# Layer one of an mLSTM and two-MoE kernel in five groups of two or three units, with two units ahead of it in place of three

## The reference

```python
m_new = np.maximum(f_gate[:, :, t] + m, i_gate[:, :, t])
f_stab, i_stab = np.exp(f_gate[:, :, t] + m - m_new), np.exp(i_gate[:, :, t] - m_new)
C = f_stab * C + i_stab * outer(v, k);  n = f_stab * n + i_stab * k
y = sigmoid(o_gate) * (C @ q) / np.maximum(np.abs(n . q), 1.0)
```

## Time and profile before

| | |
|---|---|
| median of 3 runs | 929.63 us (929.35 to 931.27) |
| the profiled execution, its own time | 928.55 us |
| its span | 926.7 us |
| PE busy | 917.5 us (99%) |
| VectorE, ACT, POOL busy | 622.0, 435.9, 621.6 us |
| mean granted clock | 0.996 |

### The profile page before, as it was taken

The page is one execution under the profiler, slowest core; times in us unless marked ns, Lnnn a source line. Parts: engine busy times, 40 slices in busy tenths (PEclk is TensorE's granted clock), DMA queues, the critical chain, the costliest instruction groups (busy, mean ns, idle before and its releaser), DMA issues.

```text
span 926.7 us, 16315 instructions
## 1 busy us (share of the span) xinstructions
PE 917.5 (99%) x6081; PEld 904.5 (98%) x6081; DVE 622.0 (67%) x1194; ACT 435.9 (47%) x887; POOL 621.6 (67%) x639
## 2 busy tenths in 40 slices
PE   9899999999999999999999999999999999999998
PEld 7799999999999999999999999999999999999998
DVE  7767555557867887866666666666666666666665
ACT  4544434326664444545445454444454444444442
POOL 5875454643877667677777767777776777677652
PEclk9899999999999999999999999999999999999999
DMA  9824204201111111111111111121111112111102
GB/s 291 254 65 114 71 26 115 78 1 38 37 38 38 38 37 39 38 38 40 57 39 52 38 38 37 38 60 38 52 37 38 38 38 56 42 51 39 37 2 86
DMA packets 28238, 53.54 MB, mean 58 GB/s; under 512 B 2288, under 2 KB 16224, under 8 KB 27776
## 3 DMA queue, kind: packets, MB, share of 16 engines
q1 hardware_dynamic: 27008, 46.73, 17.5%
q10 hardware_dynamic: 1152, 5.77, 1.6%
HBM read 50.45 MB, written 2.05 MB: 57 GB/s over the span
## 4 chain that ended last, share of the span: by engine, by line
PE 93%; DMA 2%; DVE 2%; SPq 1%; issue 0%; ACT 0%; POOL 0%; DVEq 0%; POOLq 0%
PE bank L1659 36%; PE bank L1636 33%; PE bank L1516 9%; PE bank L1526 6%; PE bank L1530 3%; PE bank L1441 2%; DMA rw<-rows 1%; PE bank L1376 1%; PE bank L1435 1%; DMA factors<-dec 1%; PE bank L1414 1%; PE bank L1548 1%; SPq L425 1%; PE bank L1431 0%; DVE acc L1277 0%
## 5 line engine op out<-in xcount | busy, mean ns | idle before, releaser
L1636 PE MATMUL bank<-xo,wu 128*128 128x384 f32 (+1 forms) x1792 | 377.4, 338 | 0.7 <-DVE s L1297 0.5
L1636 PEld LDWEIGHTS bank<-xo,wu 128*128 128x128 f32 (+1 forms) x1792 | 306.6, 188 | 1.4 <-DVE s L1297 0.7
L1281 DVE SCALAR_TENSOR_TENSOR acc<-bank,prob,acc 128x320 f32<-128x320 f32 x336 | 184.7, 550 | 143.2 <-PE bank L1659 141.7
L1659 PE MATMUL bank<-wd_hi,h_hi 128*128 128x320 f32 x768 | 232.7, 311 | 0.1
L1659 PE MATMUL bank<-wd_lo,h_hi 128*128 128x320 f32 x768 | 231.3, 309 | 0.0
L741 POOL TENSOR_TENSOR h_lo<-r,h_hi 128x384 fp32r<-128x384 f32 x192 | 194.5, 1032 | 52.4 <-ACT r L691 52.3
L741 POOL TENSOR_TENSOR wu<-raw_up,wu 128x512 fp32r<-128x512 f32 (+1 forms) x128 | 145.6, 1168 | 103.9 <-ACT wu L499 98.6
L690 ACT ACTIVATE h_hi<-c 128x384 fp32r<-128x384 f32 x192 | 100.3, 522 | 185.4 <-DVE c L1303 142.0
L1659 PE MATMUL bank<-wd_hi,h_lo 128*128 128x320 f32 x768 | 174.9, 309 | 0.0
L1659 PEld LDWEIGHTS bank<-wd_lo,h_hi 128*128 128x128 f32 x768 | 145.0, 189 | 0.0
L1659 PEld LDWEIGHTS bank<-wd_hi,h_hi 128*128 128x128 f32 x768 | 144.7, 188 | 0.2
(11 more groups left out here) (148 smaller groups left out, 1309.4 us busy)
## 6 DMA issues: line engine op xcount, KB each, us to landing
raw_up<-ups SPq DMA_DIRECT2D x32, 512.0 KB, 3.5
raw_down<-downs SPq DMA_DIRECT2D x32, 320.0 KB, 2.9
rw<-rows SPq DMA_DIRECT2D x12, 480.0 KB, 7.7
qk_s<-qk SPq DMA_DIRECT2D x12, 416.0 KB
fb<-factors SPq DMA_DIRECT2D x9, 512.0 KB, 6.4
m_raw<-up_down ACTq DMA_DIRECT2D x2, 1440.0 KB, 9.7
result<-acc SPq DMA_DIRECT2D x12, 160.0 KB, 1.8
decb<-factors SPq DMA_DIRECT2D x18, 80.0 KB
```

The source lines that it names most:

```text
L1281: ins = stt(acc[:, unit, :], bank_, prob[:, unit, ex:ex + 1], acc[:, unit, :], ALU.mult, ALU.add)
L1636: last = mm(ring_bank(q, b), a, m, start=(i == 0 and k in (0, 1, 4)), stop=(i == len(parts) - 1), skip_group_check=True)
L1659: last = mm(ps_t[n % RING][:, 0:DM], h[half + f][:, cols], w_[w][:, f, :], start=(i == 0), stop=(i == len(parts) - 1))
```

## The change

The groups of layer one become 2, 2, 2, 3 and 3 units (`SIZES`). Only units 0 and 1 are made ahead of it; units 2 and 3 are made in group 0, 4 and 5 in group 1 (one in seven steps, `PERIODS`), 6 to 8 in group 2 and 9 to 11 in group 3 (one in five). `unit_at(g, step, f)` tells which unit has which stage in step f. Unit 2 gets its factors and decays by DMA, as the later ones: `spread_decays`, `copy_decb`, the tensor `select` and the second `turn_factors` go. `fg`, `first_f` and `dec` move into the memory of the last weight tables, so VectorE's two waits go; ACT waits instead, ahead of piece 8 (`TABLES = 8`). In group 0 `gact` isn't used: the max is written over the hidden tile in its bank, of which there are three then. The weights come in six DMAs, the last three issued later, and three pieces stand ahead of group 0, the others one in each step.

```diff
-UNIT = 5
-EARLY = 6
+SIZES = (2, 2, 2, 3, 3)
+PERIODS = (7, 7, 5, 5)
+STEPS = {7: (0, 1, 2, 4, 5, 7, 8, 9), 5: (0, 1, 2, 3, 4, 5, 6, 7)}
+SCORE, QUERY, WEIGH, HEADS, DENOM, OUTPUT, TURN, LOW = range(8)
+READY = 2
-TABLES = 12
-LOADS = (0, 2, 6, 11, FT1)
-LATE = {2: (6, 7), 3: (8,), ...}
+TABLES = 8
+LOADS = (0, 2, 4, 6, 9, 12, FT1)
+LEAD = 3
...
+    def hidden_bank(g, f):
+        n = tokens(g)
+        return ((bank[6], bank[7], bank[5])[f % 3] if g == 0 else ps_h[f % 2])[:, 0:n]
+
+    def activated(g, f):
+        return hidden_bank(0, f) if g == 0 else gact[:, f % 2, 0:tokens(g)]
...
             turn_factors()
             gates_exp(1)
             load_weights(0)
-            turn_factors(1)
+            act.wait_ge(rows_in[1], 16)
             load_weights(1)
...
             def mlp_piece_at(f):
-                for q in LATE.get(f, ()):
+                q = f + LEAD
+                if q == TABLES:
+                    act.wait_ge(f_stored, 32)
+                    act.wait_ge(dec_stored, 32)
+                    act.wait_ge(iT_ready, len(PARTS))
+                    act.wait_ge(dE_ready, 2)
+                if q < FT1:
                     mlp_piece(q)
+                if f in (1, 4):
+                    load_weights({1: 4, 4: 5}[f])
...
-            turn_lo(xa_hi, 2, ps_turn_of[2], 2 * P, xa_ready)
-            decays(1, 0, 0)
-            dve.wait_ge(f_stored, 32)
-            dve.wait_ge(dec_stored, 32)
...
+                    for j in range(2):
+                        if f >= j and unit_at(g, SCORE, f - j) is not None:
+                            u = unit_at(g, SCORE, f - j)
+                            if u != STARTS[g + 1] or g == 0:
+                                decays(u, j)
+                    if g + 2 < G and f >= FT1:
+                        decays(STARTS[g + 2], f - FT1)
...
+                        if g == 0 and f >= 3:
+                            pe.wait_ge(lo1, f - 2)
+                        if g > 0 and f >= 2:
                             pe.wait_ge(g1, s - 1)
-                        first_product(ps_h[f % 2], f, ...)
+                        first_product(hidden_bank(g, f), f, ..., STARTS[g] * P, n, wait_x_lo).then_inc(h1, 1)
```

More of the change, by code:

```diff
@@ L38 @@
 PARTS = ((0, P), (P, 2 * P), (2 * P, S))
-EARLY = 6
+SIZES = (2, 2, 2, 3, 3)
+G = len(SIZES)
+STARTS = tuple(sum(SIZES[:g]) for g in range(G))
+PERIODS = (7, 7, 5, 5)
+STEPS = {7: (0, 1, 2, 4, 5, 7, 8, 9), 5: (0, 1, 2, 3, 4, 5, 6, 7)}
+SCORE, QUERY, WEIGH, HEADS, DENOM, OUTPUT, TURN, LOW = range(8)
+READY = 2
 SLOTS = 2
@@ L73, in after, with tokens, unit_at, factor_loads @@
     return m + (FREE + 1)
-def same_slot(i):
-    return (1, 3, 2)[i]
+def tokens(g):
+    return SIZES[g] * P
+def unit_at(g, step, f):
+    if g + 1 == G:
+        return None
+    for i in range(SIZES[g + 1]):
+        if i * PERIODS[g] + STEPS[PERIODS[g]][step] == f:
+            return STARTS[g + 1] + i
+    return None
+def factor_loads(u):
+    return (u - READY) // GT + 1
 NEG = -1e30
-def build(nc, gates, select, qk, rows, up_down, rest, ups, downs, wgate, consts, factors, out):
+def build(nc, gates, qk, rows, up_down, rest, ups, downs, wgate, consts, factors, out):
     f32, f32r = mybir.dt.float32, mybir.dt.float32r
@@ L205, in build @@
     mark[0] = after_x + TABLES * PM * 4
+    fg = sb("fg", [GH, S])
+    first_f = sb("first_f", [GH, S])
+    dec = sb("dec", [GH, S])
     ig = sb("ig", [GH, S])
@@ L443, in _ @@
             sp.dma_start(cst[:, :], consts).then_inc(consts_in, 16)
[L444 to L450, removed]
+            for u in range(READY):
+                load_qk(u, u)
+                load_rows(u, u)
+            load_qk(READY, READY)
+            load_rows(READY, READY)
             sp.wait_ge(f_ready, 2)
@@ L1515, in first_product, with second_product @@
                         wait_x_lo()
-                    last = mm(dst[:, 0:GN], w, x, start=(i == 0), stop=(i == len(parts) - 1))
+                    last = mm(dst, w, x, start=(i == 0), stop=(i == len(parts) - 1))
                 return last
-            def second_product(f, slot, first, last, hi, lo, wait_lo, done, wait_bank=None):
+            def second_product(f, size, slot, first, last, hi, lo, wait_lo, done, wait_bank=None):
                 col = f * PM + 2 * P
                 for w in (hi, lo):
-                    for t in range(GT):
+                    for t in range(size):
                         if first and w is hi and wait_bank is not None:
```

499 lines of the change are left out of this document (217 added, 282 removed).

## The result

The changed kernel takes **932.53 us** (median of 10 runs, 932.01 to 935.08), the kernel before, run beside it, 930.19 (10 runs). The ratio is 1.0026, with a 95% interval of 1.0014 to 1.0037: slower by 2.3 us, a little more than the 1.9 us that I named as the bound of what can be told from no change. The range held it, but the case that I gave the best chance (no difference, +0.95 us, 927.8 to 931.5) did not come. The profiled execution took 932.21 us with a span of 930.4, 3.7 us over that of before (928.55 and 926.7).

What follows compares the result with a forecast made beforehand. PE, busy in 99% of the span, was taken as the bound. The terms -7.2 - 3.7 + 4.95 + 1.4 + 2.8 + 2.2 + 0.5 gave +0.95 us on the median 929.63, so 930.6 us, range 924.0 to 936.5.

Steps and rivals of the forecast that it cites:

- the case that I gave the best chance: Whole kernel: gains and losses nearly balance, +0.95 us, 930.6 us, between 927.8 and 931.5; chance 0.36.
- Step 1: Start ahead of layer one: only two units made there, first product at about 23.8 in place of 30.96, -7.2 us.
- Step 2: Group 0: VectorE's wait on the table stores goes, and with it all 3.7 us of standing, -3.7 us.
- Step 3: Group 0: unit 2 is made there, where PE is full, +4.95 us.
- Step 4: Groups of two: first-product matmuls of 256 columns at 0.121 us each, 384 replacing 256 of 0.176, +1.4 us.
- Step 5: Group 0: PE stands for POOL's weight pieces, thirteen inside the shorter group at 1.95 us each, +2.8 us.
- Step 6: Changes of group: VectorE's max, scans and low part delay its copies; PE stands 1.2, 0.8 and 0.2, +2.2 us.
- Step 7: Group 2, three units in shorter steps: weights 0.2 to 0.4 us late for the heads twice, +0.5 us.
- third case: Group 0: POOL's weight pieces bound it, 934.5 us, last group's first product at 218; chance 0.27.
- The rival of 0.147: First-product matmuls: 256 columns cost as much as 320, 10 us more, 940.6 us; chance 0.04.
- The slower one: POOL's weight pieces bound group 0, 3 to 4 us longer, a lower clock can add; 934.5 us, chance 0.27.

Runs made afterwards that it cites:

- Run 5: Kernel before with fg, first_f and dec behind eight weight pieces and VectorE's wait on their stores gone: 930.28 us against 931.22, ratio 0.9994.
- run 6: As Run 5, with the fourth weight load issued in step 0 of group 0: 930.62 us against 931.22, ratio 0.9991.
- run 1: Changed kernel with VectorE's two scans at a change of group moved into steps 0 and 1 of the next group: 932.96 us, ratio 1.0031.
- run 12: run 9 with the scan left at the group's end held until POOL's last low part is done: 929.78 us against 930.75, ratio 0.9993.
- Run 8: Changed kernel with outputs in step 6 and a fourth weight piece made ahead of the layer: 931.35 us, ratio 1.0008.
- run 7: Changed kernel with the low part of the rest of pieces 3 to 15 made by no engine (part of result differs): 931.69 us, ratio 1.0008.
- run 9: Run 8 with one of the two scans at the group's end, the other in step 0 of the next: 930.19 us against 930.74, ratio 0.9993.
- run 3: Changed kernel with outputs and their copy in step 6 in place of 7 in groups that make two units: 931.99 us, ratio 1.0021.
- run 2: Changed kernel with the low part of the 128-row rest of pieces 3 to 15 given from POOL to VectorE: 943.95 us, ratio 1.0142.
- run 4: Changed kernel with the edits of run 1, run 2 and run 3 together: 946.69 us, ratio 1.0156.
- run 10: Run 8 with groups of two, three, two, two and three units: 945.81 us, ratio 1.0161.

## Why the prediction was right and wrong

The groups' lengths and the rows give an account that can be laid beside the prediction's sum. Work by rows is 48 steps of 1.82, 16 of 2.73 and ten units of 4.95, with 3.2 for turns and late columns: 183.8 us of the 194.67 (the 3.2 are 0.6 in group 0 and 0.87 for turns in each of the three others). Before it was 178.8 of 182.52. So the change added 5.0 of work, took 3.7 of standing away and put 10.9 there.

| Step of the prediction | predicted | measured in the profile |
|---|---|---|
| 1. start | -7.2 | -8.1 |
| 2. wait on the stores | -3.7 | -3.7 |
| 3. one more unit in the layer | +4.95 | +4.95 (taken, see below) |
| 4. 256 columns | +1.4 | 0.0 |
| 5. standing in group 0 | +2.8 | +5.1 |
| 6, 7. standing in groups 1 to 3 | +2.7 | +5.8 |
| last group's start | +0.95 | +4.0 |

The sum was too low by 5.4 us in the two rows of standing, and too high by 2.3 in the start and the 256 columns. That leaves 3.1 us in the account, and 1.9 in the time, since the forecast was laid on a median that is 1.1 us above the profiled execution. So that the range held 932.53 is in part luck: the standing was forecast at half of what it was, and other misses made up for part of it. The last group's start at 217.49 is near the 218 that the prediction gave for its third case.

- **Step 1** held: heads of unit 1 at 15.15 (predicted 15.4), first product at 22.82 (23.8). Unit 1's output ends at 21.15 (21.7), and the product follows 1.7 later (2.1 to 2.4). The long scan of `dec` takes 1.16 us where it took 2.60, with POOL no longer busy beside it. What I named only as a risk went the other way: eight of the change's ten runs have a mean clock of 1.000, and in the profiled one it stayed at 1.00 through this start, where before it fell at 24 us and, by the mean clock of most of its runs, for longer. How much of the 8.1 us the clock gave isn't measured.
- **Step 2** held in the account of the two profiles and is mis-sized by itself. Runs 5 and 6 made this part alone and it brought 0.4 to 0.9 us, with intervals that include no gain. Run 5 shows what the clamp's wait covered: PE's own wait for unit 3's keys and queries, which land at the same time with or without it. A step that I never wrote is that the profiled execution's start stands for the others. It was among the best: of the 98 runs of the kernel before beside runs 1 to 12, four had a clock of 0.996 or more, and one was faster than the profiled one. This is why the profiles differ by 3.7 us and the medians by 2.3.
- **Step 3** isn't measured by itself, and no kernel without the unit's work was tried. That group 3 has no standing, and is 59.42 long, which is 43.7 + 14.85 + 0.87, speaks for the 4.95.
- **Step 4** was mis-sized: 0.117 us a matmul, near the straight line (0.118). The fixed part that I kept for 0.121 isn't there. The Trainium skill's 262 cycles for 256 columns (TensorE: Matmul & The Clock Gate, Back-to-back issue gap) would be 0.109; the row decides. The rival of 0.147 is refuted.
- **Step 5** had the right engine and the wrong place. I had reckoned by POOL's sum of work, with piece 15 as the late one. POOL ended 0.6 us later than I said, and piece 15 was in time. The waits are at pieces 3, 4, 10 and 11, where ScalarE's rounding, a unit's stages and a meeting with a scan come together. I had taken 1.95 a piece, for fewer meetings; three small subtractions took 0.93 to 0.97 us more than alone, ahead of these waits. Run 8 removed all four waits by one piece more ahead, run 7 two of them by taking 8.8 us of subtractions. Beyond the 2.9 us of waits, each stop costs more than its idle time, which was in no term (below). With this, five stops (0.27 each) and one wait for a copy (0.3) make 4.6 of the 5.1 us; the rest isn't placed.
- **Step 6** was right in its mechanism at the first change (1.2 predicted, 0.88 in the row) and blind to the other half: the same scans hold POOL's low part, 0.82 us at the second change. The rule that I quoted for step 5 (the Trainium skill, GPSIMD Engine Reference, 1. Specifications) covers this case as well, a VectorE instruction with two SBUF inputs beside POOL, and I applied it to the pieces alone. Runs 9 and 12 show both halves: -1.1 and -0.7 in group 1.
- **Step 7** (+0.5) has 0.9 us in two waits ahead of heads in group 2. The profile names no releaser; VectorE's weights end 0.2 us ahead of both, so late weights are likely. Not foreseen were waits for ScalarE's last 64 columns before the turn of a unit (0.3 to 0.4, one in each of groups 0 to 2), which run 3 took away in groups 0 and 1.
- **The rivals.** The slower one had the right sign and cause, POOL's pieces, at 934.5, and gave the clock as what could add to it. In the change the clock did the reverse: it stayed up; in runs 2, 4 and 10 it did what the rival said. The measured time lies midway between 930.6 and 934.5. Balance was forecast since I summed the standing place by place and priced only the chains that I looked at.

## What to carry to other kernels

When a stage is filled by one engine and its steps get a third shorter, every chain through the other engines that used to be hidden comes out, one place at a time; look for them at each place where a transfer of work between engines was "just in time", and not at the engine's total. Removing one such wait pays only in part (of the 1.7 us of waits taken away in run 1, 0.4 arrived in the profile and 0.7 in the time at 1.000), and moving work to an engine with idle time can cost far more than it frees: run 2 lost 11.4 us where I had hoped for a gain of 2.5. Before a start-up stretch is priced from one profile, see whether that execution is a typical one.

## What the runs showed of the hardware

- **VectorE's scan and POOL's instructions hardly run side by side, and the delay goes in both directions.** In most rows the one that starts first goes at full speed and the other waits: `m_st` took 1.42 in place of 0.45 beside a scan that started 0.05 us earlier. A scan that starts while POOL is busy waits, and at times POOL's next instruction goes ahead of it too: the scan took 3.69 in place of 1.22 when POOL's queries had started 0.17 us earlier (run 2), and the scan of `dec` 2.60 in place of 1.16. At 43.67 in the changed kernel it took only 1.45, and POOL's next instruction was the one that waited (`m_st`, 1.39). An order that keeps them apart by a wait (run 12) is faster than one that lets them meet.
- **A stop of PE costs some 0.27 us more than its idle time.** At 94.67 in the changed kernel the row says 0.40 of idle. But the last two matmuls before it, at 0.147 each, make room for the next at 94.11, so the gap is 0.56, and the eight matmuls behind the stop take 1.04 in place of 0.93. The stops at 29.17 and 32.22 give 0.28.

```profile
93.82 0.46 PE L1505 MATMUL bank<-m_hi,ht_lo 128*128 128x320 f32 x2
94.67 0.50 PE L1491 MATMUL bank<-xt_hi,m_hi 128*128 128x256 f32 x2 [0.40 <-DVE gact L1179]
...
95.71 0.46 PE L1501 MATMUL bank<-m_hi,ht_hi 128*128 128x320 f32 x2
```

- **At a stop of PE the granted clock can fall to 0.50**, 1.2 GHz: at one of 2.92 us in run 10 (0.59 of another shortly before), at one of 4.05 in run 5, after 1.85 and 2.10 with little between them in run 2. In runs 5 and 10 it falls before the stop is over. The changed kernel's waits of at most 1.0 us in group 0 left it at 1.00. The length of the stop doesn't settle it: the kernel before stood for 3.00 us, until 35.60, and kept 1.00 (window of 32 to 36 us, clock behind the busy times), when it had been at the lower level until 31 us. That it is the standing that does it is read from the order of the rows; no run changed it alone.

```profile
32.00:36.00 4.00, 0.99 (x10) 0.68 (x10) 1.43 (x1) 1.41 (x4) 4.00 (x4) 1.00 0.72 164
```
